# Attention stage of a fused attention, dense and routed layer: the weighted products of a pair of heads in one group per three jobs, one of three weight copies on ScalarE, keys loaded in three pieces and V in one

## The chip, the cores and the metric

The kernel runs on one core of a Trainium2 chip. The metric is the device time of one launch in microseconds (us), lower is better. The core has a matrix engine (TensorE, PE in the profile, with its weight loads as PEld), a vector engine (DVE), a scalar engine (ACT), a general engine (GpSimd, POOL) and SyncE (SP), which here only issues transfers. Each engine runs its own queue in order, and engines wait for each other through semaphores.

## What is computed

Three layers follow each other; only the first is touched.

```python
# q, k, v: (4, 8, 576, 64); window 64
scores = q @ k.T / sqrt(64);  keep only 0 <= row - col < 64
attn = softmax(scores)                       # exp(x - max) / sum
x = (attn @ v) laid out as (2304, 512)
xn = x / rms(x) * rms_g
y = (silu(xn @ w_gate) * (xn @ w_val)) @ w_out     # (512 -> 1536 -> 512)
# then each row goes to the best of 8 experts: relu(y @ w1[e]) @ w2[e], gated
```

## The kernel before

The attention is done in 16 units (`UNITS`), a unit being one pair of heads of one batch. A unit has nine blocks of 64 rows (`NBLK`), each against 128 keys, and they are done three at a time: a job is three blocks, a unit three jobs (b = 0, 1, 2), 48 jobs in all. The two heads of a pair lie side by side: each block's queries are laid out with zeros (`lay_out_q`, on GpSimd) so that one 128-row product makes the scores of both heads.

For job j the work passes through the engines as follows.

- TensorE, `scores`: one mask product (L922) and six score products recorded in L928 (two entries per product) into the bank of b. It waits until the exponentials of job j-3 are done, and at the first job of a unit for queries and keys.
- VectorE, `row_max` (L1262); ScalarE, `exps` (L692): three exponentials, each with its row sum read back; VectorE, `normalize` (L1270 reciprocal, L1272 product) of the job before.
- TensorE, `weights_T` (L945): three transposes of job j-3, into one of two banks in turn; VectorE, `copy_pt` (L1278), copies them to `pt`.
- TensorE, `weighted` (L957): for job j-4, 12 entries of L957 (three blocks, two heads) into one of two output banks in turn; ScalarE, `copy_o` (L702), copies them to `xo`.

So PE's queue holds, for each job: mask, scores, transposes, weighted products. DVE's: maximum, copy of transposes, normalize. ACT's: exponentials, copy of outputs.

SyncE's queue loads, unit by unit: `load_q` of unit n+2, the first piece of V of unit n, `load_k` of unit n+1 (it waits until all scores of unit n-1 are done), two more pieces of V, and `store_xT` of unit n-2, which waits for ScalarE's copies. A unit moves 288 KB each of q, k and output, and 512 KB of V, whose windows overlap. Beside it come strips of the dense weights (`load_dense` on ScalarE's queue before pairs 3, 5 and 7, 1 MB each).

GpSimd lays out the queries of the next unit and between them splits weight strips into a high and a low part, squares the first chunk of x (units 10 and 11), scales it (`scale_first`: quarters 0 and 1 at n = 14, quarters 2 and 3 at n = 15, after `lay_out_q(n)`) and splits it (`split_first`). The scale waits for the inverse roots, which go through ScalarE (`root_first`, with the table for square roots, then `copy_first_roots`, L765, after pair 6), VectorE (at jobs 1 and 2 of pair 6) and TensorE (`token_mean_squares` before unit 12, `spread_first_roots` in the last job of unit 13).

After job 47, `attention_end` mixes the last transposes and weighted products with the first gate products (`half_gate`, L1000 to L1002), which wait quarter by quarter for `split_first`. Then the dense stage runs, bound by TensorE.

```python
def job(j, i, u, b):                       # DVE, before
    row_max(j, u, b)
    copy_pt(*job_before(j, i, T_LAG))
    normalize(*job_before(j, i, 1))
```

Of the kernel before, what the change touches and what calls it, by code (L numbers as in the profile page):

```python
# [29 lines left out]
P = 128  # L30
# [11 lines left out]
T_LAG, O_LAG = 3, 4  # L42
# [79 lines left out]
def build(nc, qT, kT, vW, w_gate, w_val, w_out, rms_g, wg2, wg2T, w1, w2, out):  # L122
# [18 lines left out]
    with ExitStack() as ctx:  # L141
# [138 lines left out]
        k_in = [sem(f"k_in{u}") for u in range(2)]  # L280
        v_in = [[sem(f"v_in{u}_{b}") for b in range(JOBS)] for u in range(2)]
# [3 lines left out]
        q_first, k_first, qbd_first = sem("q_first"), sem("k_first"), sem("qbd_first")  # L285
# [24 lines left out]
        exp_ready, pt_copied, o_copied = sem("exp_ready"), sem("pt_copied"), sem("o_copied")  # L310
# [8 lines left out]
        def job_before(j, i, lag):  # L319

            i = (i - lag) % (2 * JOBS)
            return j - lag, i // JOBS, i % JOBS

        def windows(b):

            return slice(max(BPJ * b - 1, 0), BPJ * (b + 1) - 1)
# [30 lines left out]
        def _(sp):  # L357
            sp.dma_start(qraw[0][:, FIRST], qT[0][:, FIRST]).then_inc(q_first, 16)
            sp.dma_start(qraw[0][:, REST], qT[0][:, REST]).then_inc(q_in[0], 16)
            sp.dma_start(kt[0][:, REST], kT[0][:, REST]).then_inc(k_in[0], 16)  # L360
# [10 lines left out]
            def load_k(n, u):  # L371
                sp.wait_ge(s_ready, done(JOBS * (n - 1)))
                sp.dma_start(kt[u][:], kT[bass.ds(n, 1)].rearrange("a p s -> p (a s)")).then_inc(k_in[u], 16)

            def load_v(n, u, b):
                sp.wait_ge(o_ready, done(JOBS * (n - 2) + b + 1))
                sp.dma_start(vt[u][:, windows(b), :].rearrange("p j c -> p (j c)"),
                             vW[bass.ds(n, 1), :, windows(b), :].rearrange("a p j c -> p (a j c)")
                             ).then_inc(v_in[u][b], 16)

            def store_xT(n, u):
                sp.wait_ge(o_copied, done(JOBS * (n + 1)))
# [12 lines left out]
            load_k(1, 1)  # L395
            for u in range(2):
                for b in range(JOBS):
                    load_v(u, u, b)
            load_q(2, 0)
            load_q(3, 1)  # L400
            load_k(2, 0)

            def unit(n, u, q=True, k=True):
                if q:
                    load_q(n + 2, u)
                load_v(n, u, 0)
                if k:
                    load_k(n + 1, 1 - u)
                load_v(n, u, 1)
                load_v(n, u, 2)  # L410
                store_xT(n - 2, u)
# [13 lines left out]
            unit(UNITS - 1, 1, q=False, k=False)  # L425
            load_wo(1)
# [15 lines left out]
            sp.wait_ge(o_ready, done(STEPS))  # L442
# [1237 lines left out]
```

## Time and profile before

| | us |
|---|---|
| median of 3 runs (838.75 to 839.33) | 838.92 |
| the profiled execution | 838.17 |
| its span | 836.2 |
| attention, first work to first gate product of f = 1 | up to 105.6 |
| TensorE busy | 820.1 (98%) |
| VectorE busy | 484.2 |
| ScalarE busy | 287.1 |
| GpSimd busy | 211.9 |

The granted clock of TensorE is full in all 40 slices of the page. In the first five slices (104 us) VectorE is 6 to 8 tenths busy, ScalarE 5 to 7, and the DMA engines 7 to 9 tenths; after that TensorE is nearly alone.

### The profile page before, as it was taken

To read this page: it belongs to the slowest core of one execution; us is meant where nothing else is said; L and a number is where in the kernel's file an instruction comes from. 1 tells how busy PE (TensorE), PEld (TensorE's weight loads), DVE (VectorE), ACT (ScalarE), POOL (GpSimd) and SP (SyncE) were. 2 spreads that over 40 slices of the span, in tenths; PEclk is the share of its full clock that TensorE was granted. 3 is DMA by queue.
4 is the path that set the end of the run, shared out by engine and by line. 5 is a ranking of instruction groups with operands and counts; after the bars stand their busy time and mean duration, and the time that the engine had idled before them with its cause. 6 is when DMAs were issued, how large, how long until landed. Compare 5 with 4: busy or idle time off the path is not lost.

```text
span 836.2 us, 15281 instructions
## 1 busy us (share of the span) xinstructions
PE 820.1 (98%) x4809; PEld 732.6 (88%) x4810; DVE 484.2 (58%) x994; ACT 287.1 (34%) x665; POOL 211.9 (25%) x187
## 2 busy tenths in 40 slices
PE   8999999999999999999999999999999999999996
PEld 7888799999999998999999999998888888888885
DVE  7888632548675865676485767735224645564351
ACT  6777521321212121212213123334315435444340
POOL 4276899303002100300030000050831111111100
PEclk9999999999999999999999999999999999999999
DMA  7898970010002000200100012216354544646100
GB/s 233 266 312 273 326 303 1 1 44 33 1 1 76 0 1 4 76 0 1 55 22 1 1 39 101 101 39 225 96 208 151 189 175 151 225 180 216 53 17 23
DMA packets 38888, 88.24 MB, mean 106 GB/s; under 512 B 4063, under 2 KB 13791, under 8 KB 38305
## 3 DMA queue, kind: packets, MB, share of 16 engines
q1 hardware_dynamic: 33632, 72.79, 25.3%
q0 software_dynamic: 3360, 10.23, 3.4%
q10 hardware_dynamic: 1824, 4.31, 1.6%
q8 instruction: 40, 0.66, 0.3%
q14 instruction: 32, 0.25, 0.1%
HBM read 73.16 MB, written 14.94 MB: 105 GB/s over the span
## 4 chain that ended last, share of the span: by engine, by line
PE 95%; POOL 2%; DVE 1%; ACT 1%; issue 1%; DMA 1%; ACTq 0%; POOLq 0%; DVEq 0%
PE ps L1000 27%; PE ps L1002 27%; PE ps L1001 27%; PE ps L928 3%; PE ps L1138 2%; PE ps L957 2%; PE ps L922 2%; PE ps L945 1%; PE ps L1059 1%; ACT pr L692 1%; POOL xn_lo L551 0%; POOL xc L543 0%; PE ps L1175 0%; DVE nmax L1262 0%; PE ps L903 0%
## 5 line engine op out<-in xcount | busy, mean ns | idle before, releaser
L1000 PE MATMUL ps<-xn_hi,GV_hi 128*128 128x384 f32 x576 | 195.7, 340 | 1.1 <-POOL xn_lo L551 0.7
L1001 PE MATMUL ps<-xn_lo,GV_hi 128*128 128x384 f32 x576 | 193.0, 335 | 0.8 <-issue 0.8
L1002 PE MATMUL ps<-xn_hi,GV_lo 128*128 128x384 f32 x576 | 193.4, 336 | 0.0
L1000 PEld LDWEIGHTS ps<-xn_hi,GV_hi 128*128 128x128 f32 x576 | 108.2, 188 | 5.4 <-POOL xn_lo L551 1.0
L1001 PEld LDWEIGHTS ps<-xn_lo,GV_hi 128*128 128x128 f32 x576 | 108.2, 188 | 3.3
L1002 PEld LDWEIGHTS ps<-xn_hi,GV_lo 128*128 128x128 f32 x576 | 108.1, 188 | 0.9 <-issue 0.9
L1359 DVE CUSTOM_DVE_ANT_0 ps<-ysb,wrb 128x512 f32<-128x512 f32 x120 | 92.1, 768 | 6.0 <-ACT ysb L756 1.0
L743 ACT ACTIVATE sig<-ps 128x384 f32<-128x384 f32 x72 | 35.4, 492 | 168.7 <-PE ps L1002 168.6
L749 ACT ACTIVATE h_hi<-ps 128x384 fp32r<-128x384 f32 x72 | 35.4, 491 | 166.7 <-DVE ps L1329 166.7
L1002 PE MATMUL ps<-Wo_hi,h_lo 128*128 128x512 f32 x216 | 85.5, 396 | 0.0
L1001 PE MATMUL ps<-Wo_lo,h_hi 128*128 128x512 f32 x216 | 85.3, 395 | 0.0
L1324 DVE TENSOR_TENSOR silu<-sig,ps 128x384 f32<-128x384 f32 x72 | 39.8, 552 | 77.2 <-ACT sig L743 73.8
L1000 PE MATMUL ps<-Wo_hi,h_hi 128*128 128x512 f32 x216 | 84.1, 389 | 0.3 <-issue 0.3
L1000 PE MATMUL ps<-EW_hi,h2T_hi 128*128 (+1 forms) x168 | 67.2, 400 | 1.1 <-DVE osb L1564 1.1
L1000 PE MATMUL ps<-EW_hi,xsT_hi 128*128 (+1 forms) x168 | 68.0, 405 | 0.0
L626 POOL DMA_INDIRECT out<-osb,sidx x21 | 21.1, 1004 | 182.1 <-DVE osb L1564 181.6
L559 POOL TENSOR_TENSOR ssq<-xraw 128x384 f32<-128x384 f32 x5 | 5.6, 1115 | 240.5 <-DMA xraw<-xT_rows 240.5
L1002 PE MATMUL ps<-EW_hi,xsT_lo 128*128 (+1 forms) x168 | 66.5, 396 | 0.0
L1001 PE MATMUL ps<-EW_lo,xsT_hi 128*128 (+1 forms) x168 | 66.3, 395 | 0.0
L1329 DVE TENSOR_TENSOR ps<-silu,ps 128x384 f32<-128x384 f32 x72 | 40.5, 563 | 44.3 <-PE ps L1002 43.0
L1002 PE MATMUL ps<-EW_hi,h2T_lo 128*128 (+1 forms) x168 | 65.7, 391 | 0.0
L1001 PE MATMUL ps<-EW_lo,h2T_hi 128*128 (+1 forms) x168 | 65.7, 391 | 0.0
(176 smaller groups left out, 1393.2 us busy)
## 6 DMA issues: line engine op xcount, KB each, us to landing
EW_raw<-w SPq DMA_DIRECT2D x32, 1024.0 KB, 7.1
vt<-vW SPq DMA_DIRECT2D x32, 192.0 KB, 4.4
xT_rows<-xo SPq DMA_DIRECT2D x16, 288.0 KB, 4.0
y_rows<-ysb SPq DMA_DIRECT2D x6, 768.0 KB, 4.1
qraw<-qT SPq DMA_DIRECT2D x15, 288.0 KB, 4.0
kt<-kT SPq DMA_DIRECT2D x15, 288.0 KB, 4.7
xraw<-xT_rows SPq DMA_DIRECT2D x5, 768.0 KB, 5.6
vt<-vW SPq DMA_DIRECT2D x16, 128.0 KB, 4.3
```

Of the source, the lines that this page charges most:

```text
L626: nc.gpsimd.indirect_dma_start(out=out, out_offset=bass.IndirectOffsetOnAxis(ap=sidx[:, s:s + 1], axis=0), in_=osb[s % DEEP][:], in_offset ...
L743: nc.scalar.activation(sig[:], ps[:, G_BANK + f % 2, 0:CH], ACT.Sigmoid).then_inc(sig_ready, 1)
L749: nc.scalar.activation(h_hi[f % 2][:], ps[:, V_BANK + f % 2, 0:CH], ACT.Copy).then_inc(hi_ready, 1)
L922: return nc.tensor.matmul(ps[:, S_BANK + b, 0:BPJ * KEYS], ident_r[:], masks, start=start, stop=not start)
L928: last = nc.tensor.matmul(ps[:, S_BANK + b, i * KEYS:(i + 1) * KEYS], qbd[u][:, k, :], kt[u][:, k0:k0 + KEYS], start=(start and i == 0), s ...
L957: last = nc.tensor.matmul(ps[half, O_BANK + (JOBS * u + b) % 2, i * WIN:(i + 1) * WIN], vt[u][:, max(k - 1, 0), half], pt[:, b, i * P + a ...
L1000: nc.tensor.matmul(out, a_hi, b_hi, start=start, stop=False)
L1001: nc.tensor.matmul(out, a_hi, b_lo, start=False, stop=False)
L1002: return nc.tensor.matmul(out, a_lo, b_hi, start=False, stop=stop)
L1324: nc.vector.tensor_tensor(silu[:], sig[:], ps[:, G_BANK + f % 2, 0:CH], ALU.mult).then_inc(silu_ready, 1)
L1329: nc.vector.tensor_tensor(hid, silu[:], hid, ALU.mult).then_inc(h_ready, 1)
L1359: v.tensor_tensor_reduce(out=ps[:, MISC, :], in0=ysb[:, t, :], in1=wrb[:, e, :], scale=1.0, scalar=0.0, op0=ALU.mult, op1=ALU.add, accum_o ...
```

## The change

The order of work within a unit changes; no arithmetic does.

- `weighted` becomes one call per unit: 36 entries of L957 for unit n-2, in the first job of unit n, after the first transposes of unit n-1. It waits for all three copies of the transposes, for the V of the unit, and for `normalize` of job (n-1, 1).
- `weights_T` of unit n-1, job b is done in job b of unit n.
- Of the three copies of transposed weights, ScalarE makes the third (`move_pt`, ahead of the exponentials of b = 2). VectorE's two wait for the weighted products of the unit before.
- `copy_o` becomes one copy of 128x576 per unit, after the exponentials of b = 0.
- The reciprocals of b = 1 go to the second output bank; this `normalize` waits for `copy_o`, and the next `weighted` waits for this `normalize`.
- Keys come in three transfers per unit with a semaphore each, V in one. SyncE's order is q, three pieces of k, V, store. The first piece of k may start one job earlier.
- The third strip of dense weights is loaded by SyncE after the last unit's loads, no longer by ScalarE before pair 7.
- All four quarters of `scale_first` come at n = 15, after `lay_out_q(15)`. `attention_end` has a new order, and the last `normalize` uses another bank.

```diff
-T_LAG, O_LAG = 3, 4
+O_LAG = 2
@@ sync
-            def load_k(n, u):
-                sp.wait_ge(s_ready, done(JOBS * (n - 1)))
-            def load_v(n, u, b):
-                sp.wait_ge(o_ready, done(JOBS * (n - 2) + b + 1))
+            def load_k(n, u, b):
+                sp.wait_ge(s_ready, done(JOBS * (n - 2) + min(b + 2, JOBS)))
+            def load_v(n, u):
+                sp.wait_ge(o_ready, done(n - 1))
             def store_xT(n, u):
-                sp.wait_ge(o_copied, done(JOBS * (n + 1)))
+                sp.wait_ge(o_copied, done(n + 1))
...
+            load_strip(2)
             load_wo(1)
             load_strip(3)
@@ gpsimd
-            scale_at = {14: (0, 1), 15: (2, 3)}
+            scale_at = {15: range(KD)}
@@ scalar
+            def move_pt(n, u):
+                act.wait_ge(pt_ready, done(JOBS * n + JOBS))
+                act.wait_ge(o_ready, done(n))
+                nc.scalar.activation(pt[:, JOBS - 1, :], ps[:, T_BANK + (JOBS * u + JOBS - 1) % 2, 0:BPJ * P],
+                                     ACT.Copy).then_inc(pt_moved, 1)
+            def copy_o(n, u, stored):
+                act.wait_ge(o_ready, done(n + 1))
+                act.wait_ge(xT_out[u], stored)
+                nc.scalar.activation(xo[u][:], ps[:, O_BANK:O_BANK + 2, :].rearrange("p a c -> p (a c)")[:, 0:S],
+                                     ACT.Copy).then_inc(o_copied, 1)
...
+                for j, u, b in jobs(2 * JOBS * pair, 2 * JOBS):
+                    if b == JOBS - 1:
+                        move_pt(2 * pair + u - 1, 1 - u)
                     exps(j, u, b)
+                    if b == 0:
+                        copy_o(2 * pair + u - O_LAG, u, 16 * pair)
...
-            load_dense(2)
@@ tensor
+            def weighted(n, u, loads, normalized):
+                pe.wait_ge(pt_copied, done(2 * n + 2))
+                pe.wait_ge(pt_moved, done(n + 1))
+                pe.wait_ge(v_in[u], loads)
+                pe.wait_ge(o_copied, done(n))
+                pe.wait_ge(p_ready, normalized)
+                for k in range(NBLK):
...
+                    weights_T(n - 1, 1 - u, b)
+                    if b == 0:
+                        weighted(n - O_LAG, u, 16 * pair, done(JOBS * (n - 1) + 2))
...
             def attention_end(c, par):
+                weights_T(UNITS - 1, 1, 0)
+                pe.wait_ge(exp_ready, done(STEPS - JOBS + 1))
+                half_gate(c, 0, par, *gv_weights[0], range(0, 1))
+                weighted(UNITS - 2, 0, 8 * UNITS, done(STEPS - 1))
+                weights_T(UNITS - 1, 1, 1)
+                half_gate(c, 0, par, *gv_weights[0], range(1, KD))
+                weights_T(UNITS - 1, 1, 2)
                 pe.wait_ge(exp_ready, done(STEPS))
                 half_gate(c, 0, par, *gv_weights[1])
+                weighted(UNITS - 1, 1, 8 * UNITS, done(STEPS))
@@ vector
+            def normalize(n, u, b, bank=None):
+                j, blocks = JOBS * n + b, slice(b * BPJ, (b + 1) * BPJ)
+                if b == 1:
+                    dve.wait_ge(o_copied, done(n - 1))
+                    bank = O_BANK + 1
...
+            def normalize_last(n, u, b):
+                if b == 0:
+                    normalize(n - 1, 1 - u, JOBS - 1)
+                else:
+                    normalize(n, u, b - 1)
+            def copy_pt(n, u, b):
+                dve.wait_ge(pt_ready, done(JOBS * n + b + 1))
+                dve.wait_ge(o_ready, done(n))
...
+            def job(j, n, u, b):
                 row_max(j, u, b)
+                if b < JOBS - 1:
+                    copy_pt(n - 1, 1 - u, b)
+                normalize_last(n, u, b)
```

## Rows read from the trace of the kernel before

**Rows 1.** Page, part 1: busy time, share of the span, instructions.

```profile
PE 820.1 (98%) x4809; PEld 732.6 (88%) x4810; DVE 484.2 (58%) x994; ACT 287.1 (34%) x665; POOL 211.9 (25%) x187
```

**Rows 2.** Busy time by stretch: engines (instructions), PE clock, DMA share, GB/s.

```profile
30.50:36.10 5.60, 5.60 (x70) 4.89 (x66) 5.00 (x13) 4.13 (x22) 1.46 (x3) 1.00 0.84 262
41.70:47.50 5.80, 5.75 (x70) 4.89 (x66) 5.09 (x13) 4.21 (x22) 4.96 (x5) 1.00 1.02 376
```

**Rows 3.** Timeline of PE, unit 6: start, duration, engine, line, operation, count.

```profile
37.06 0.49 PE L945 MATMUL ps<-ident,pr 128*128 128x128 f32 x3
37.48 0.57 PE L957 MATMUL ps<-pt,vt 128*64 128x64 f32 x12
37.98 0.44 PE L922 MATMUL ps<-mask,ident_r 128*128 128x384 f32 x1
38.26 0.83 PE L928 MATMUL ps<-kt,qbd 128*128 128x128 f32 x6
```

**Rows 4.** Timeline of PE, jobs 3 and 4, before any weighted products.

```profile
8.83 0.42 PE L922 MATMUL ps<-mask,ident_r 128*128 128x384 f32 x1
...
10.00 0.42 PE L922 MATMUL ps<-mask,ident_r 128*128 128x384 f32 x1
```

**Rows 5.** Timeline of DVE, job 5, where it runs without a gap.

```profile
13.49 0.55 DVE L1262 TENSOR_REDUCE nmax<-ps 128x3 f32<-128x384 f32 x1
...
13.96 0.55 DVE L1278 COPY pt<-ps 128x384 f32<-128x384 f32 x1
...
14.42 0.17 DVE L1270 RECIPROCAL ps<-den 128x3 f32<-128x3 f32 x1
...
14.63 0.55 DVE L1272 TENSOR_TENSOR pr<-pr,ps 128x384 f32<-128x384 f32 x1
...
15.10 0.55 DVE L1262 TENSOR_REDUCE nmax<-ps 128x3 f32<-128x384 f32 x1
```

**Rows 6.** Timeline of ACT: exponentials of one job, its copies of 192 and 384 columns.

```profile
70.07 0.37 ACT L692 ACTIVATE pr<-ps,nmax 128x128 f32<-128x128 f32 x1 [0.49 <-DVE nmax L1262]
...
71.11 0.33 ACT L702 ACTIVATE xo<-ps 128x192 f32<-128x192 f32 x1
...
109.18 0.49 ACT L749 ACTIVATE h_hi<-ps 128x384 fp32r<-128x384 f32 x1 [1.29 <-DVE ps L1329]
```

**Rows 7.** Timeline of PE: first mask products of units 9 and 15, with idle time.

```profile
54.20 0.43 PE L922 MATMUL ps<-mask,ident_r 128*128 128x384 f32 x1 [1.03 <-ACT pr L692]
...
90.76 0.45 PE L922 MATMUL ps<-mask,ident_r 128*128 128x384 f32 x1 [0.52 <-POOL qbd L521]
```

**Rows 8.** Timeline of SP: issue of the keys of unit 9.

```profile
48.37 0.33 SPq L373 DMA_DIRECT2D kt<-kT  x1
```

**Rows 9.** Page, part 6: transfers, KB each, median us from issue to landing.

```profile
kt<-kT SPq DMA_DIRECT2D x15, 288.0 KB, 4.7
```

**Rows 10.** Timeline of PE before unit 12: the mean squares.

```profile
72.06 0.83 PE L910 MATMUL ps<-ones_r,ssq 128*128 128x1 f32 x6
```

**Rows 11.** Timeline of ACT in unit 12: first table load, next exponential.

```profile
73.33 1.28 ACT L760 ACT_TABLE_LOAD   x1
...
76.19 0.37 ACT L692 ACTIVATE pr<-ps,nmax 128x128 f32<-128x128 f32 x1
```

**Rows 12.** Timeline of ACT: the inverse roots copied out.

```profile
85.27 0.50 ACT L765 ACTIVATE ssq<-ps 128x384 f32<-128x384 f32 x1
```

**Rows 13.** Timeline of POOL after the roots: queries of unit 15, last split.

```profile
89.24 1.47 POOL L521 TENSOR_SCALAR qbd<-qraw,heads 128x576 f32<-128x576 f32 x2
...
99.27 1.00 POOL L551 TENSOR_TENSOR xn_lo<-xc,xn_hi 128x384 fp32r<-128x384 f32 x1
```

**Rows 14.** Timeline of PE: end of the attention, first gate product of f = 1.

```profile
100.33 0.45 PE L1000 MATMUL ps<-xn_hi,GV_hi 128*128 128x384 f32 x1 [0.69 <-POOL xn_lo L551]
...
105.14 0.57 PE L957 MATMUL ps<-pt,vt 128*64 128x64 f32 x12
105.64 0.45 PE L1000 MATMUL ps<-xn_hi,GV_hi 128*128 128x384 f32 x1
```

More of the change, by code:

```diff
@@ L394, in _ @@
             load_q(1, 1)
-            load_k(1, 1)
+            for b in range(JOBS):
+                load_k(1, 1, b)
             for u in range(2):
-                for b in range(JOBS):
-                    load_v(u, u, b)
+                load_v(u, u)
             load_q(2, 0)
             load_q(3, 1)
-            load_k(2, 0)
+            for b in range(JOBS):
+                load_k(2, 0, b)
             def unit(n, u, q=True, k=True):
@@ L405, in unit @@
                     load_q(n + 2, u)
-                load_v(n, u, 0)
                 if k:
-                    load_k(n + 1, 1 - u)
-                load_v(n, u, 1)
-                load_v(n, u, 2)
+                    for b in range(JOBS):
+                        load_k(n + 1, 1 - u, b)
+                load_v(n, u)
                 store_xT(n - 2, u)
@@ L771, in _ @@
             act.dma_start(raw_out[0][:].rearrange("p k d -> p (k d)"), w_out[0]).then_inc(wo_in[0], 16)
-            load_dense(2)
             with act.Fori(STRIP_PAIRS[2], UNITS // 2) as pair:
                 pair_of_units(pair)
-            for i in range(O_LAG):
-                copy_o(*job_before(STEPS + i, i, O_LAG), 16 * (UNITS // 2))
+            copy_o(UNITS - 2, 0, 8 * UNITS)
+            move_pt(UNITS - 1, 1)
+            copy_o(UNITS - 1, 1, 8 * UNITS)
             def round_part(e, i):
@@ L1004, in _, with half_gate @@
             gv_weights = ((0, G_BANK, g_ready), (1, V_BANK, v_ready))
-            def half_gate(c, f, par, kind, bank, ready):
+            def half_gate(c, f, par, kind, bank, ready, ks=range(KD)):
                 strip, cols = f // FPS, slice(f % FPS * P, (f % FPS + 1) * P)
-                for k in range(KD):
+                for k in ks:
                     if f == 0:
@@ L1012, in half_gate @@
                                  (xn_hi[par][:, k, :], xn_lo[par][:, k, :]), k == 0, k == KD - 1)
-                last.then_inc(ready, 1)
+                if ks[-1] == KD - 1:
+                    last.then_inc(ready, 1)
             def gate_val(c, f, par, between=None):
@@ L1027, in sum_y @@
                 if first and f == 0:
-                    pe.wait_ge(o_copied, done(STEPS))
+                    pe.wait_ge(o_copied, done(UNITS))
                 if f == 0:
@@ L1302, in _ @@
                                             sq[:, 0:TPC].unsqueeze(2).to_broadcast([P, TPC, P]), ALU.mult).then_inc(first_diag, 1)
-            for i in range(T_LAG):
-                copy_pt(*job_before(STEPS + i, i, T_LAG))
-                if i == 0:
-                    normalize(*job_before(STEPS, 0, 1))
+            dve.wait_ge(rrms_ready, done(1))
+            normalize(UNITS - 1, 1, JOBS - 1, MISC)
+            for b in range(JOBS - 1):
+                copy_pt(UNITS - 1, 1, b)
             def norm_rows(c, k, par):
```

116 lines of the change are left out of this document (41 added, 75 removed).

## The prediction

> **What bounds the kernel now.** I read the busy times first [rows 1]: PE is busy for 98% of the span, so time is saved only where PE's queue gets shorter or where PE waits. The change touches the attention alone, up to the first gate product of f = 1 at 105.64 [rows 14]; behind it nothing changes, and the dense stage needs GpSimd's weight strips some us before PE uses them, so what the attention gains is the kernel's gain. Second, busy time by stretch: in a quiet unit PE is busy in all of its 5.60 us, DVE in 5.00, ACT in 4.13 [rows 2]. So PE is the bound of a unit, DVE is close behind, and a change that lightens PE meets DVE next. Third, PE's timeline within a job [rows 3]: transposes at 37.06, weighted products at 37.48, mask at 37.98, scores at 38.26. A third of 5.60 is 1.87 a job. Last, the waits of PE: the first mask of unit 9 comes after 1.03 idle [rows 7], and there is a second like it at unit 11; the page names ACT, but those exponentials were long done, and it was the keys: issued at 48.37 [rows 8], they took up to 5.5 us to land, over their median of 4.7 [rows 9], behind a stretch with the DMA share at 1.02 and 376 GB/s [rows 2]. Unit 15 waits 0.52 for GpSimd's layout of queries [rows 7].
>
> **PE's own work after.** With its 12 weighted products a job takes 1.87. Without any, the masks of jobs 3 and 4 stand at 8.83 and 10.00 [rows 4]: 1.17. So a group of 12 costs 0.70. Its merged row is 0.57 long [rows 3], of which the last product is about 0.27, so the starts of 11 take 0.30: 0.028 for each. 12 x 0.028 = 0.34 is streaming, and 0.36 is the change over from transposes and to the mask. One group of 36 costs 36 x 0.028 + 0.36 = 1.37 where three cost 2.10. PE's unit falls from 5.60 to 2 x 1.17 + (1.17 + 1.37) = 4.88.
>
> **DVE's own work.** Where it runs without a gap [rows 5], the maximum takes 0.47 to the next start, the copy 0.46, reciprocal 0.21, product 0.47: 1.61 a job, 4.83 a unit. ACT takes one copy of three, so DVE has 4.37. ACT: exponentials 1.04 from first to the copy behind them [rows 6], three times 3.12; the copy of 384 columns took 0.49 and of 192 took 0.33 [rows 6], so one of 576 should take 0.65 (an estimate by these two); 3.12 + 0.49 + 0.65 = 4.26. By work alone PE would still be the bound, at 4.88.
>
> **The new wait.** But the products of unit n-2 (first job of unit n) wait for `normalize` of job (n-1, 1), and DVE's first copy in that job waits for the products. This closes a ring through both queues, once a unit. From the copy's start on DVE: copy 0.46, reciprocal 0.21, product 0.47 (job 2 of the unit before); maximum 0.47, copy 0.46, reciprocal 0.21, product 0.47 (b = 0); maximum 0.47, reciprocal 0.21, product to its end 0.56 (b = 1). That is 3.99 [rows 5]. Then PE: 0.06 from a release to a start (as from 100.27 to 100.33, [rows 13, 14]), 35 x 0.028 + 0.27 = 1.25 for the products, 0.05 to DVE. Sum 5.35. It is longer than PE's 4.88, so I take 5.35 as the unit: PE waits some 0.47 in front of the weighted products of each unit, and the gain per unit is 0.25, not 0.72. Only the maximum of b = 0 runs beside the products. Queued behind the waiting products is the mask of b = 1; behind DVE's waiting copy the whole rest of its unit.
> I walked the other queues past the ring, from the start W of the products: scores of b = 1 are ready at W + 2.29 and DVE wants them at 2.44; those exponentials end at 4.1 and their reciprocal comes at 4.53; `move_pt` ends by 4.6 and is wanted at 5.35. None is in the ring, the tightest has 0.15.
>
> **Up to the roots.** In job 5 the maximum starts at 13.49 in both; after, the reciprocal follows at once and its product ends at 13.49 + 0.47 + 0.21 + 0.56 = 14.73, so the first group of 36 starts at 14.79 in unit 2. Unit 13's starts 11 rings later: 14.79 + 58.85 = 73.6. Onto this come:
> - Table loads. From 73.33 to 76.19 [rows 11], 2.86 us, ACT does no exponentials. Before, this hid in ACT's slack. After, the exponentials of unit 11 end at W + 0.37, so those of (12, 0) start at 3.23, copy of outputs by 4.95, (12, 1) ends at 6.0, and the normalize in the ring starts at 6.05 and ends at 6.82 instead of 5.30: +1.5. Where this cover is partly there it costs nothing, at worst 2.9. The Trainium skill ("ScalarE: Activation LUTs", section What ACT_TABLE_LOAD costs) gives about 2.66 us for a switch to another set, drain included; the row's 2.86 holds two loads and a small root, so by the page's figure for both switches the cost would be up to 5.3. The trace decides for less.
> - Mean squares, up to 0.83 on PE [rows 10] before unit 12, and a like pair for the spread in unit 13: before both were paid in full, now 0.47 of each lies in PE's wait: +0.2 for the first; the second comes behind the roots' path in part.
> - Transfers. The first keys may be asked for 1.2 earlier and the other pieces are wanted 1 to 2 jobs later, while V, stored outputs and queries have 6 us and more. So the stalls of units 9 and 11 (1.0 each) and 0.2 at unit 8 should go. Bounds: 0 to 2.2 left; I take 0.5, since a unit's traffic (1.41 MB) is now spread over 5.35, and three units with strip and chunk (6.07 MB) at the 376 GB/s of [rows 2] need 16.1, just 3 x 5.35. A piece has 96 KB instead of 288, V 512 instead of three pieces: packets of a unit stay as many.
> Unit 13's products start at 73.6 + 1.5 + 0.2 + 0.5 = 75.8. The exponentials of (13, 2) end 5.7 later, the copy of the roots 0.5 after that: 82.1, where before it was 85.77 [rows 12]. Gain 3.7.
>
> **From the roots to the end.** GpSimd goes from 85.77 to 100.27 = 14.5 [rows 12, 13] without a gap, and this includes the layout of unit 15, 1.47 [rows 13] less a small overlap, now done before the roots: 13.1 is left, its last split ends at 95.2. PE reaches its last gate quarter at about 95.0, so the split stays last. From 100.27 to 105.64 [rows 13, 14] lie three groups of 12 and two of transposes; after there is one of transposes and one of 36: 3 x 0.50 + 0.42 go, about 1.15 comes, 5.37 - 0.8 = 4.6. Gate products of f = 1 at 99.8. Gain 105.64 - 99.8 = 5.8 to 5.9. Moving strip 2 to SP: GpSimd wants it only after its first split of w_out, which begins at 95.2; issued near 88, it has over 7 us before that even begins (288 KB take 4.7, [rows 9]). It costs 0.
>
> **Sum.** Profiled execution 838.17 - 5.9 = 832.3. The median of the runs is 0.75 above that execution: 833.0.
>
> **Rivals.**
> B. The ring doesn't bind, PE does (the release comes earlier than by my rows, or DVE pipelines its steps closer). 11 units at 4.88 instead of 5.35: 5.2 less, of which PE's insertions take 0.5: 828. For it: the margin is only 0.47 in 5.35. Against: every step of the ring is a row.
> C. Slower. The transfers become the bound. Place: units 6 to 14, 9 x 1.41 + 2.9 = 15.6 MB, hidden in 9 x 5.35 = 48 us at 324 GB/s. The quiet unit moved 262 at a share of 0.84, which is 312 at a full share: 50, costing 1.8. It decides from 15.6 MB / (48.2 + 5.9) = 288 GB/s on: below that all is lost. At 280 it is 55.7, 7.5 lost: 840.5. Against it: 376 was moved in one stretch. The Trainium skill ("DMA: Bandwidth & Descriptors", section Bandwidth) calls for transfers of 1 MiB and puts those under 64 KB down to descriptors; pieces of 96 KB go that way. By it C would gain weight; it changes no term above.
> D. The ring passes every disturbance on. Before, a late key, a table load or a late layout met slack in three queues; now each meets 0.15 to 0.5. If the 2.2 of key stalls stay and the table loads cost 2.9, the gain is 5.9 - 1.7 - 1.4 = 2.8: 836.
> E. The ring is longer than 5.35 and reaches 5.60 (0.25 more, for example by exponentials that come in late): 11 x 0.25 = 2.8 lost, with D's terms nothing is left: 839.
>
> **How the numbers follow.** Forecast 0.50, B 0.14, C 0.09, D 0.20, E 0.07. Its own range is 831 to 835. The range to hold 8 in 10 takes in B's edge and D: 828.0 to 837.8. A measurement here tells 0.2%, 1.7 us, from no change. Faster by more (below 837.2): the forecast, B and most of D, 0.81. Within it: E and the end of D, 0.09. Slower: C and a bad E, 0.10.
>
> **What would show it.** Right: L957 in 16 merged groups of 36 of about 1.25; mask to mask of b = 0 every 5.35 in quiet units; PE idle for 0.4 to 0.5 ahead of L957, released by DVE L1272's line; DVE idle in front of the copy of b = 0, released by L957; one longer unit of about 6.9 at unit 12 to 13, with ACT's table loads; no idle in front of the masks of units 9 and 11; POOL without a gap from the roots for 13.1. Wrong: units of 4.9 (B), units above 5.5 with the DMA share near 1 and keys or V released by DMA (C), POOL not ready.

## The result and the profile after

| us | before | after |
|---|---|---|
| median (lowest to highest) of 9 runs each | 838.75 (836.79 to 840.25) | 836.74 (834.96 to 837.63) |
| profiled execution, its span | 838.17, 836.2 | 836.86, 834.9 |
| first gate product of f = 1 | 105.64 | 104.76 |

The ratio is 0.9970, with an interval of 0.9959 to 0.9981: some 2.5 us faster, where 5.9 were forecast. A second, later set of 8 runs of the changed kernel gave 835.19 and a ratio of 0.9957 (0.9937 to 0.9976). So the change is a gain, but of 5.9 us only 2.5 to 3.6 arrived. In the profiled executions the attention gave 0.88, and the part behind it 0.42.

That small remainder hides two larger things. TensorE stops once near 330 us for a reason that the profile doesn't name ("issue"), and longer after the change. The second row of each pair is the same place of the program, the router's products, some 235 us later; first before, then after:

```profile
331.40 0.34 PE L1001 MATMUL ps<-xn_lo,GV_hi 128*128 128x384 f32 x1 [0.77 <-issue]
...
565.51 2.85 PE L1167 MATMUL ps<-wr,yT_last 128*128 128x8 f32 x24
```

```profile
330.79 0.33 PE L1005 MATMUL ps<-xn_hi,GV_lo 128*128 128x384 f32 x1 [1.51 <-issue]
...
565.83 2.85 PE L1171 MATMUL ps<-wr,yT_last 128*128 128x8 f32 x24
```

So there the changed kernel is 0.32 behind. What puts it 1.3 ahead at the end is, by the rows, a spell at half clock right behind these products, worth 1.7, that the profile of before has and that of after has not (last section). That the change gains rests on the two sets of runs, not on this pair of profiles.

The page of after: busy times, and two of the transfers (KB each, median us to landing):

```profile
PE 810.5 (97%) x4809; PEld 729.5 (87%) x4810; DVE 474.9 (57%) x978; ACT 291.3 (35%) x649; POOL 211.9 (25%) x187
...
vt<-vW SPq DMA_DIRECT2D x16, 512.0 KB, 4.8
...
kt<-kT SPq DMA_DIRECT2D x47, 96.0 KB, 4.1
```

PE's busy time fell by 9.6 us against [rows 1], much more than the span, which fell by 1.3: PE does less, and waits for most of what it saved. The timeline of PE in after, the group of 36 weighted products in the first job of units 2 to 13 (two quiet ones and unit 10 left out) (start, duration, idle time ahead and its releaser), shows where:

```profile
16.86 1.98 PE L967 MATMUL ps<-pt,vt 128*64 128x64 f32 x36
22.95 1.27 PE L967 MATMUL ps<-pt,vt 128*64 128x64 f32 x36 [0.38 <-DVE pr L1282]
28.31 1.27 PE L967 MATMUL ps<-pt,vt 128*64 128x64 f32 x36 [0.38 <-DVE pr L1282]
...
44.41 1.27 PE L967 MATMUL ps<-pt,vt 128*64 128x64 f32 x36 [0.38 <-DVE pr L1282]
51.08 1.27 PE L967 MATMUL ps<-pt,vt 128*64 128x64 f32 x36
57.69 1.27 PE L967 MATMUL ps<-pt,vt 128*64 128x64 f32 x36
...
68.42 1.27 PE L967 MATMUL ps<-pt,vt 128*64 128x64 f32 x36 [0.39 <-DVE pr L1282]
75.02 1.27 PE L967 MATMUL ps<-pt,vt 128*64 128x64 f32 x36
80.90 1.27 PE L967 MATMUL ps<-pt,vt 128*64 128x64 f32 x36 [0.89 <-DVE pr L1282]
```

Quiet units take 28.31 - 22.95 = 5.36, with 0.38 of waiting for the DVE product: that is the ring. But unit 2 starts late and its group lasts 1.98, and the groups of units 8, 9 and 12 come 6.67, 6.61 and 6.60 behind the ones ahead of them. What stands ahead of them on PE, in four stretches of the same timeline:

```profile
14.66 0.44 PE L925 MATMUL ps<-mask,ident_r 128*128 128x384 f32 x1 [1.93 <-POOL qbd L517]
...
49.72 0.43 PE L925 MATMUL ps<-mask,ident_r 128*128 128x384 f32 x1 [1.49 <-DMA kt<-kT]
...
56.33 0.44 PE L925 MATMUL ps<-mask,ident_r 128*128 128x384 f32 x1 [1.44 <-DMA kt<-kT]
...
73.68 0.41 PE L925 MATMUL ps<-mask,ident_r 128*128 128x384 f32 x1 [0.88 <-issue]
```

These are the first masks of units 2, 8, 9 and 12; such waits were forecast to go. The last three wait for keys (at 73.68 the profile names none; it goes when the keys come earlier, below). SyncE's queue in after, ahead of unit 8, tells why (start, duration of the issue), behind ScalarE's copy of outputs:

```profile
40.86 0.65 ACT L703 ACTIVATE xo<-ps 128x576 f32<-128x576 f32 x1
...
41.95 0.41 SPq L378 DMA_DIRECT2D xT_rows<-xo  x1
42.65 0.40 SPq L364 DMA_DIRECT2D qraw<-qT  x1
43.24 2.04 SPq L369 DMA_DIRECT2D kt<-kT  x3
```

The keys stand behind the store, and the store waits for ScalarE's copy of outputs, which now is one copy late in the job (40.86 to 41.51). So they are asked for at 43.24 and would be wanted at 49.72 - 1.49 = 48.23. Call this distance their lead, 5.0 here, and compare it with how long after the issue PE could start on them:

| first keys, us | before | after | `store_late` (below) |
|---|---|---|---|
| lead, units 5, 6, 7 | 5.6, 5.9, 5.7 | 4.8, 5.0, 4.8 | 6.3, 6.2, 6.3 |
| unit 8: lead, mask behind the issue | 6.1, no wait | 5.0, 6.5 | 6.5, 6.7 |
| unit 9 | 4.8, 5.8 | 5.5, 6.9 | 6.4, no wait |
| unit 11 | 5.4, 6.4 | 4.6, no wait | 6.3, no wait |
| unit 12 | 7.6, no wait | 5.4, 6.3 | 7.0, 7.3 |

The change was to bring the keys 1.2 earlier. Of the units in this table only unit 9 got more lead, 0.7; the others got 0.7 to 2.2 less. In units 8, 9 and 12 the keys then came 6.3 to 6.9 after their issue (before, the slowest of units 9 and 11 took 6.4), so a lead of 5.0 to 5.5 was not enough.

### The profile page after: what moved, and what is told of

Its sections match the earlier page's. It is cut to its first block, busy times and chain, and to the rows that moved or that the text cites. A ratio compares the mean times of both kernels' runs of the same rounds, so it can differ in the third digit from the quotient of the medians.

```text
span 834.9 us, 15300 instructions
## 1 busy us (share of the span) xinstructions
PE 810.5 (97%) x4809; PEld 729.5 (87%) x4810; DVE 474.9 (57%) x978; ACT 291.3 (35%) x649; POOL 211.9 (25%) x187
## 4 chain that ended last, share of the span: by engine, by line
PE 90%; DVE 3%; issue 3%; ACT 2%; DMA 1%; POOL 1%; SPq 0%; DVEq 0%; ACTq 0%; POOLq 0%
PE ps L1003 27%; PE ps L1005 27%; PE ps L1004 27%; PE ps L1142 2%; PE ps L967 2%; PE ps L1063 1%; ACT pr L688 1%; DVE nmax L1266 1%; DMA kt<-kT 1%; DVE pr L1282 1%; DVE pt L1295 1%; PE ps L931 1%; PE ps L1179 0%; DVE ps L1280 0%; PE ps L951 0%
```

## The experiments

The ratios are to the kernel before, run on the same chip, with 95% intervals; its medians there were 838.12 to 838.73. "Group of unit n" is the start of the 36 products that PE does in the first job of unit n. Each kernel has one profile, and two profiles of one kernel differ too (`after_again`, below), so the rows show where time goes and the ratios how much of it counts. Line numbers shift by a few from kernel to kernel.

### Order of SyncE's queue

`store_late`: the same transfers with the same waits, only that each store moves behind the queries and keys that stood behind it.

```diff
 def unit(n, u, q=True, k=True):
-    if q: load_q(n + 2, u)
-    if k: load_k(n + 1, 1 - u, b)      # three pieces
     load_v(n, u)
+    if q: load_q(n + 3, 1 - u)
+    if k: load_k(n + 2, u, b)          # three pieces
     store_xT(n - 2, u)
```

> The changed kernel with SyncE's order in a unit turned: V of n, queries of n+3, keys of n+2, and only then the store of unit n-2. The first keys no longer stand behind a store that waits for ScalarE's output copy. Theory SyncE order: keys are issued about 1.5 us earlier relative to their unit, the idle of PE ahead of the first masks of units 8, 9 and 12 (1.49, 1.44, 0.88) goes, the distances of 6.6 there fall to about 5.4, and the kernel gains 3 to 3.8 us. Rival (the DMA engines are simply full there): the landing moves with the load, units 8 and 9 keep over 1 us each, gain under 1 us.

Measured: 833.29 (832.68 to 834.26), ratio 0.9955 (0.9939 to 0.9972). SyncE and PE in store_late around unit 8:

```profile
40.19 2.01 SPq L369 DMA_DIRECT2D kt<-kT  x3
42.67 0.36 SPq L378 DMA_DIRECT2D xT_rows<-xo  x1
...
46.92 0.44 PE L930 MATMUL ps<-mask,ident_r 128*128 128x384 f32 x1 [0.26 <-DMA kt<-kT]
```

The keys of unit 8 are issued 6.5 ahead of their demand and still take 6.7, so it is the lead that helps, not a faster landing. The waits for keys are 0.26, 0.18 and 0.22 (units 8, 10 and 12) where they were 1.49, 1.44 and 0.88 (units 8, 9 and 12). The groups of units 8 and 9 come after 5.42 and 5.37. The place of the store was the cause of the waits. From unit 12 to 13 it now takes 6.55 where after had 5.88, so part of the gain is given back to the table loads, which the late keys had covered. By the ratio alone the edit can't be told from after (0.9970 and 0.9957): the 3 to 3.8 us that I expected are seen in the rows, not in the time.

`start_v1_late`: at the start, V of unit 1 is loaded behind the queries and keys of unit 2 instead of ahead of them.

```diff
-            for u in range(2):
-                load_v(u, u)
+            load_v(0, 0)
             load_q(2, 0)
             load_q(3, 1)
             for b in range(JOBS):
                 load_k(2, 0, b)
+            load_v(1, 1)
```

> The changed kernel, with the V of unit 1 (wanted at 20 us) issued after the queries of units 2 and 3 and the keys of unit 2. Theory start: the queries of unit 2, which landed at 12.9, land at about 11, PE's idle of 1.93 ahead of unit 2 and the slow clock behind it go, the first group of 36 starts near 14.8 instead of 16.86 and the second at 20.2 instead of 22.95: 2 to 2.8 us less. Rival (the queries were late for the total of bytes): the idle stays over 1 us, gain under 1 us.

Measured: 833.77 (833.06 to 836.44), ratio 0.9957 (0.9943 to 0.9972). GpSimd's layout of unit 2's queries, first in after, then in start_v1_late:

```profile
12.95 2.91 POOL L517 TENSOR_SCALAR qbd<-qraw,heads 128x576 f32<-128x576 f32 x4 [3.26 <-DMA qraw<-qT]
```

```profile
10.71 1.47 POOL L517 TENSOR_SCALAR qbd<-qraw,heads 128x576 f32<-128x576 f32 x2 [1.03 <-DMA qraw<-qT]
```

Both kernels issue these queries at the same time (5.85 and 5.84), but they land 2.2 earlier when no V of unit 1 is under way ahead of them. The first group starts at 14.93 (forecast 14.79; after 16.86). The waits at units 8, 9 and 12 stay (1.56, 0.60, 1.60). How much this is worth differs from execution to execution: in the eight profiles of kernels that issue as after does up to there, GpSimd starts this layout between 11.49 and 12.96 and the first group comes between 14.87 (`after_no_switch`) and 16.86 (after itself); in the four with V of unit 1 behind, it is 10.51 to 10.98 and 14.19 to 14.93. So the V ahead does hold the queries back, by 0.5 to 2.5, but the start in the profile of after is the latest of the eight, and the ratio doesn't tell this kernel from after.

`store_and_start`: both edits together.

> Both SyncE edits together: the store of unit n-2 behind the keys of unit n+2, and the V of unit 1 behind the keys of unit 2. By the traces of each alone (groups of 36 start 1.1 us earlier at unit 2 with the second, and lose 0.2 instead of 3.8 us at units 8, 9, 12 with the first), the last group should start near 98.4 and the time be 831 to 832.5, some 6 us below the kernel before: the size that was predicted for the change. Rival: the start is lost again in the full stretch, 833.

Measured: 832.24 (831.58 to 833.86), ratio 0.9917 (0.9896 to 0.9938). Groups of units 2, 3, 11, 12 and 13, and the first gate product of f = 1 in store_and_start:

```profile
14.64 1.27 PE L972 MATMUL ps<-pt,vt 128*64 128x64 f32 x36 [0.52 <-DVE pr L1287]
20.00 1.27 PE L972 MATMUL ps<-pt,vt 128*64 128x64 f32 x36 [0.38 <-DVE pr L1287]
...
62.91 1.27 PE L972 MATMUL ps<-pt,vt 128*64 128x64 f32 x36 [0.38 <-DVE pr L1287]
68.49 1.27 PE L972 MATMUL ps<-pt,vt 128*64 128x64 f32 x36
75.39 1.27 PE L972 MATMUL ps<-pt,vt 128*64 128x64 f32 x36 [1.05 <-DVE pr L1287]
...
99.28 0.45 PE L1008 MATMUL ps<-xn_hi,GV_hi 128*128 128x384 f32 x1
```

The ratio is clear of that of after in the first set of runs (0.9959 to 0.9981) and touches that of the second (0.9937 to 0.9976). This is the timeline that was forecast: a start at 14.64 (14.79), units of 5.36 (5.35), 5.58 over the mean squares (+0.2), 6.90 over the table loads (6.9), unit 13 at 75.39 (75.8) and the gate at 99.28 (99.8). The forecast time was 833.0. (Of the 6.4 gained over before at that place 0.8 is lost again up to the router's products, most of it at the stop near 330, which is 1.20 long here.)

### The ring

`rden_sbuf_free`: the reciprocals are written over the row sums in SBUF instead of into a PSUM bank, so that neither VectorE nor the weighted products need the waits that protect the bank.

```diff
-                if b == 1:
-                    dve.wait_ge(o_copied, done(n - 1))
...
-                rden = ps[:, bank, RDEN_AT:RDEN_AT + BPJ]
+                rden = den[u][:, blocks]
...
-                pe.wait_ge(p_ready, normalized)
```

> The changed kernel, with the reciprocals of the row sums written over the row sums in SBUF instead of into a PSUM bank; the wait of the weighted products for `normalize` and that of `normalize` for the output copy are gone. Theory ring: in quiet units the distance of two groups of 36 weighted products falls from 5.37 to PE's own 4.88, about 0.45 per unit in 8 or 9 undisturbed units, so 3 to 4 us less than the changed kernel, if no keys are later for it. Rival (DVE's own work or late transfers bound the unit): 5.2 to 5.4 stays, within 0.5 us of the changed kernel. If the operand in SBUF made DVE's product slower or faster than 0.56, the rows will show it.

Measured: 840.56 (838.44 to 842.90), ratio 1.0041 (1.0016 to 1.0066): slower. The ring is open, since groups come every 4.91 (15.38, 20.30, 25.22, 30.13, 35.04) with no wait ahead of them, and PE's own 4.88 of the forecast is right. But new costs come. GpSimd and VectorE in rden_sbuf_free, two layouts with the product of `normalize` beside them:

```profile
28.86 2.21 POOL L517 TENSOR_SCALAR qbd<-qraw,heads 128x576 f32<-128x576 f32 x2 [2.69 <-PE ps L931]
...
28.81 0.56 DVE L1276 TENSOR_TENSOR pr<-pr,den 128x384 f32<-128x384 f32 x1
...
29.96 0.59 DVE L1276 TENSOR_TENSOR pr<-pr,den 128x384 f32<-128x384 f32 x1
```

The pair of layouts takes 2.21, where it took 1.47. And the next keys don't hold the pace: the mask of unit 7 waits 1.35 for them at 40.20. The larger cost comes from unit 7 on, where GpSimd splits weight strips beside the units: VectorE's product is held until GpSimd's instruction is over. GpSimd and VectorE in rden_sbuf_free:

```profile
66.59 2.54 POOL L527 TENSOR_TENSOR GV_lo<-GV_raw,GV_hi 128x1024 fp32r<-128x1024 f32 x1
...
67.96 1.59 DVE L1276 TENSOR_TENSOR pr<-pr,den 128x384 f32<-128x384 f32 x1
```

The 48 products take 852 ns on average where they take 554 in after, 14.3 us of DVE in all, and PE's transposes wait 4.8 for them. The group of unit 13 comes at 79.16, only 1.7 before that of after, and 2.65 of lead had been there at unit 3 (20.30 against 22.95). I expected 3 to 4 us less than after; it is slower than before.

`rden_sbuf_wait`: the same, but the wait of the weighted products for `normalize` stays.

> As the kernel before it in this list, but the weighted products still wait for `normalize` of the job (n-1, 1), though nothing needs it. It parts the wait from the place of the reciprocals. Theory ring: the distance stays at 5.37 and the time at that of the changed kernel, within 0.5 us. Rival (the place in PSUM was the cost): 4.9, as without the wait.

Measured: 842.61 (841.51 to 844.42), ratio 1.0070 (1.0052 to 1.0088). The period is 5.39 again (15.29, 20.68, 26.07, 31.45, 36.84), with 0.40 idle released by the DVE product. It is the wait that makes the ring, not the place of the reciprocals. The place costs time all the same: I expected the time of after within 0.5, and it is some 6 slower, with the same held products (747 ns on average).

`ring_open`: the reciprocals of b = 1 go to another PSUM bank (`MISC`, unused up to unit 11), and up to there the weighted products don't wait for `normalize`.

```diff
-                if b == 1:
+                if b == 1 and early[0]:
+                    bank = MISC
+                elif b == 1:
                     dve.wait_ge(o_copied, done(n - 1))
                     bank = O_BANK + 1
...
-                pe.wait_ge(p_ready, normalized)
+                if normalized is not None:
+                    pe.wait_ge(p_ready, normalized)
...
+            pe.wait_ge(p_ready, done(2 * JOBS * MS_PAIR - 1))
             token_mean_squares()
```

> The changed kernel with the reciprocals of b = 1 in the bank MISC up to unit 11, where nobody else uses it, so that neither `normalize` nor the weighted products wait there; the operand stays in PSUM, unlike in the two kernels with it in SBUF. Theory ring: the distance is 4.9 in units 2 to 6, with GpSimd's layout at its old 0.74 per instruction, not 1.11. From unit 7 on the keys are later by what was gained (they stand behind the store), so PE waits over 2 us for them in places and most of the gain is lost: 0 to 2 us less than the changed kernel. Rival (ring was the cost): 3 us less or more.

Measured: 836.10 (832.08 to 840.16), ratio 0.9964 (0.9943 to 0.9985), the same as after. Groups come every 4.91 (22.07, 26.98, 31.90, 36.81), and the layouts take 1.47. Then PE in ring_open meets what comes next:

```profile
41.99 0.43 PE L925 MATMUL ps<-mask,ident_r 128*128 128x384 f32 x1 [1.36 <-POOL qbd L517]
...
55.47 0.44 PE L925 MATMUL ps<-mask,ident_r 128*128 128x384 f32 x1 [2.24 <-ACT pr L688]
```

In after's order of SyncE's queue a shorter unit only reaches the late transfers sooner. The edit has a cost of its own too: the last line of the cut hands the bank back, and PE waits 1.56 there, at 73.58. Unit 13 is at 81.53, later than after's 80.90.

`ring_open_all`: the ring open and both edits of SyncE's order.

> Ring open up to unit 11, and both SyncE edits. Theory, transfers bind next: ten units at 4.9 instead of 5.37 would give 4 to 4.7 us over the two SyncE edits alone, but 6.07 MB in units 6 to 8 need 16.1 us at the 376 GB/s seen, so those stay near 5.4; 1.5 to 3 us less than the two edits alone, 829 to 830.5. Rival (transfers hide): 827.5. Rival (it collides with GpSimd's strips or the roots): no gain, 832.

> Ring open up to unit 11 and both SyncE edits, the same kernel again: 830 to 831.5, a ratio of 0.990 to 0.992 to the kernel before.

Measured: 830.81 (830.37 to 833.15), ratio 0.9904 (0.9883 to 0.9925); on another chip 831.62 (829.72 to 832.29), ratio 0.9921 (0.9903 to 0.9939). It is the fastest kernel of the study, 7 to 8 us below before and 4 to 6 below after. Its waits, on PE in ring_open_all:

```profile
43.15 0.43 PE L930 MATMUL ps<-mask,ident_r 128*128 128x384 f32 x1 [0.59 <-ACT pr L693]
...
53.90 0.44 PE L930 MATMUL ps<-mask,ident_r 128*128 128x384 f32 x1 [0.67 <-DMA kt<-kT]
...
65.54 0.83 PE L918 MATMUL ps<-ones_r,ssq 128*128 128x1 f32 x6 [1.56 <-DVE pr L1293]
```

Its group of unit 11 is at 60.18, 2.7 ahead of that of store_and_start, and seven of the units up to there take 4.91 or 4.92. The last wait, in front of the mean squares, is where my edit hands the bank back; it costs most of what unit 12 had gained (67.58 against 68.49), but the table loads hide behind it, and unit 13 is 2.2 ahead (73.17 against 75.39). By the medians the ring was worth 1.4 us (832.24 to 830.81) once the transfers came in time, with intervals that overlap (0.9896 to 0.9938 and 0.9883 to 0.9925); in the rows it is 2.2 at unit 13. I had expected 1.5 to 3.

### Table loads

`after_no_switch` and `before_no_switch`: the square root of the mean squares is replaced by an exponential, in after and in before, so that ScalarE loads no other table. Both kernels leave out the right root.

```diff
-                nc.scalar.activation(sq[:, 0:TPC], ps[:, MISC, 0:TPC], ACT.Sqrt, bias=eps[:],
+                nc.scalar.activation(sq[:, 0:TPC], ps[:, MISC, 0:TPC], ACT.Exp, bias=eps[:],
```

> The changed kernel with an exponential in place of the square root of the first chunk, so that ScalarE loads no other table in unit 12; this leaves the right root out, so the first chunk's scale is not that of the reference. Table loads of 2.86 us. Theory of the prediction (loads cost 1.5 us in the ring): with the keys of unit 12 late besides, the group of unit 13 comes 5.37 after that of unit 12 instead of 5.88; 0.5 to 1.5 us less than the changed kernel. Rival (ScalarE's slack hides them): same within 0.3.

> The kernel before with an exponential in place of the square root of the first chunk, so without the two table loads; the right root is left out. Theory: before, ScalarE's slack hid them, so the time stays within 0.5 us of the kernel before. Rival (they cost as in the ring): 1 to 1.5 us faster.

Measured: 834.56 (833.69 to 840.99), ratio 0.9958 (0.9930 to 0.9985), and 838.90 (836.95 to 842.57), ratio 1.0010 (0.9993 to 1.0026). From the group of unit 12 to that of 13 it takes 5.59 in after_no_switch instead of after's 5.88. But start_v1_late, which has the loads, takes 5.59 too. So where PE has waited for keys and the exponentials are ahead, the loads cost 0 to 0.3, and the time can't be told from after's. In store_and_start, where the keys are in time, this unit takes 6.90, 1.3 over the 5.59; that the loads are the cause there is argued from the rows, as no run takes them out of that kernel. Before they cost nothing that can be seen. ACT in after:

```profile
74.26 1.28 ACT L763 ACT_TABLE_LOAD   x1
75.56 0.26 ACT L763 ACTIVATE sq<-ps,eps 128x3 f32<-128x3 f32 x1
75.84 1.28 ACT L688 ACT_TABLE_LOAD   x1
77.13 0.37 ACT L688 ACTIVATE pr<-ps,nmax 128x128 f32<-128x128 f32 x1
```

Two switches with the root between take 2.87, as they did before [rows 11]. By the Trainium skill ("ScalarE: Activation LUTs", section What ACT_TABLE_LOAD costs) each would be 2.66, 1.38 of it drain; these rows show its 1.28 for the load, and no drain: the next instruction starts 0.02 behind its end.

### Size of the pieces

`keys_one`: after, with the keys of a unit in one transfer, which waits as before the change until all three jobs of the unit two before are scored. `v_three`: after, with V in three transfers. `v_three_keys_one`: both.

```diff
# keys_one
-                sp.dma_start(kt[u][:, job_cols(b)], kT[bass.ds(n, 1), :, job_cols(b)]...)
+                if b == 0:
+                    sp.wait_ge(s_ready, done(JOBS * (n - 1)))
+                    sp.dma_start(kt[u][:], kT[bass.ds(n, 1)]...)
# v_three
-                sp.dma_start(vt[u][:]..., vW[bass.ds(n, 1)]...)
+                for b in range(JOBS):
+                    js = slice(max(BPJ * b - 1, 0), BPJ * (b + 1) - 1)
+                    sp.dma_start(vt[u][:, js, :]..., vW[bass.ds(n, 1), :, js, :]...)
```

> The changed kernel with the keys of a unit in one transfer from unit 1 on, which waits until unit n-1 is scored and which the first scores of a unit wait for. It tells what the three pieces are worth. Theory: SyncE reaches the keys only behind the store anyway, so the earlier wait of the first piece is worth nothing, but a piece of 96 KB lands before 288 KB do: with one transfer PE idles longer ahead of units 8, 9 and 12 by 0 to 0.7 each, 0.5 to 1.5 us slower than the changed kernel. Rival (pieces cost more issue time and smaller packets than they bring): equal or faster by up to 1.

> The changed kernel with V in three transfers as before, still waiting for the group of 36 of unit n-2. Theory (one V of 512 KB holds back what is issued behind it): the queries of unit 2 land near 11 again, PE's idle ahead of unit 2 is under 0.6, and the first group of 36 starts at 14.8 to 15.2. Rival (the pieces of V do not matter, the place in the queue does): 14.9 to 16.9 as in the changed kernel, and PE's idle of 0.5 to 1.5 at units 8, 9 and 12 as there.

> V in three and the keys in one transfer, all transfers as before but for what they wait for. If pieces matter at the start, here the queries of unit 2 land at 10.7 to 11. If not, the start is as late as with keys in one alone, 15.2, and the time 835 as there.

Measured: keys_one 835.04 (833.49 to 839.99), ratio 0.9963 (0.9946 to 0.9981); v_three 840.89 (838.23 to 845.70), 1.0041 (1.0017 to 1.0064); v_three_keys_one 837.55 (835.38 to 846.44), 0.9993 (0.9968 to 1.0019).

keys_one equals after, against my expectation of 0.5 to 1.5 slower: three pieces of keys are worth nothing that can be measured, though the last is wanted two jobs after the first. V in one transfer, on the other hand, matters: with V in three the kernel is slower than before. With keys in one besides, the loss is smaller (0.9993), and its interval overlaps that of keys_one. SyncE at the start of v_three and PE's longest wait there:

```profile
4.61 2.80 SPq L375 DMA_DIRECT2D vt<-vW  x6
7.46 0.90 SPq L364 DMA_DIRECT2D qraw<-qT  x2
...
58.05 0.43 PE L927 MATMUL ps<-mask,ident_r 128*128 128x384 f32 x1 [3.29 <-DMA kt<-kT]
```

Six issues of V take 2.80 of SyncE's queue, where two took 0.91 (4.61 to 5.52), and all that stands behind them is that much later. I had expected the queries to land near 11, as the sizes go; they landed at 13.61. The Trainium skill ("DMA: Bandwidth & Descriptors", section Bandwidth) calls for large transfers. v_three agrees with it in direction; for keys of 96 KB against 288 no difference shows. Which of the two counts more for v_three, bytes under way or time in the queue, these runs don't separate.

### Place of the scale

`scale_split`: after, with quarters 0 and 1 of `scale_first` ahead of the layout of unit 15 again, as before.

```diff
-            scale_at = {15: range(KD)}
+            scale_at = {14: (0, 1), 15: (2, 3)}
```

> The changed kernel with the first two quarters of `scale_first` back at unit 14, ahead of the layout of unit 15. In the changed kernel GpSimd waits 1.44 for the roots after that layout. Theory: the layout of 1.47 stands in the path again, so the last split and the end of the attention come 1.4 later, and unit 15 may wait for its queries: 1.4 to 2.4 us slower than the changed kernel. Rival (PE is later than the splits at the end): within 0.5.

Measured: 837.21 (834.70 to 842.56), ratio 0.9993 (0.9970 to 1.0016). The layout comes at 87.35, behind two quarters, and PE in scale_split waits for it:

```profile
88.87 0.44 PE L925 MATMUL ps<-mask,ident_r 128*128 128x384 f32 x1 [2.02 <-POOL qbd L517]
```

From the group of unit 13 to the first gate product of f = 1 it takes 25.33 where after takes 23.86, so the new place is worth 1.5 in the rows. By the medians it is 2 against after on the same chip (837.21 and 835.19, `after_again`) and 0.5 against the first set of after (836.74). The intervals overlap in both cases; the wait itself is in the row, and after has none there.

`after_again`: the changed kernel unaltered.

> The changed kernel itself once more, for its start. In its first profile the queries of unit 2 landed at 12.9 and PE's clock was granted at half for 3.4 us behind the idle time; the first group of 36 started at 16.86. In the kernel without table loads, whose start is the same code, it started at 14.87. Theory: the start is at the edge and differs from execution to execution by up to 2 us; this profile shows a start between 14.8 and 17, and the keys of units 8, 9 and 12 late again by 0.5 to 1.5 each. Rival: the start is always 16.9.

Measured: 835.19 (833.24 to 837.13), ratio 0.9957 (0.9937 to 0.9976). Its waits for keys are 0.82, 0.73 and 1.51, its first group is at 16.55. The late start and the three waits come again, with other sizes. Not in every execution: the same start code gave a first group at 14.87 in after_no_switch and 15.15 in scale_split.

## Why the prediction was right on the ring and wrong on the transfers

In the profiled execution the miss at the first gate product (104.76 instead of 99.8) lies ahead of the group of unit 13, at 80.90 instead of 75.8. Behind it, roots, splits and the end of the attention took 23.86 (80.90 to 104.76) where 24.0 were forecast.

| up to unit 13's group, us | forecast | after | store_and_start |
|---|---|---|---|
| start of unit 2's group | 14.79 | 16.86 | 14.64 |
| first unit behind it, over 5.35 | 0 | 0.74 | 0.01 |
| quiet units | 5.35 | 5.36 | 5.36 |
| stalls for keys, units 8, 9, 12 (forecast: in all) | 0.5 | 1.31, 1.25, 1.0 | under 0.1 |
| mean squares | 0.2 | 0.2 | 0.2 |
| unit 12 to 13 (table loads), over 5.36 | 1.5 | 0.52 | 1.54 |
| unit 13's group | 75.8 | 80.90 | 75.39 |

- **Right: the ring.** Forecast 5.35 and a wait of 0.47; measured 5.36 and 0.38. rden_sbuf_free and ring_open take the wait away and show PE's own 4.91 (forecast 4.88). Rivals B and E are out.
- **Right: the small terms.** The copy of 576 columns takes 0.65, the tail from roots to last split 12.9 (13.1), the end from there 4.40 (4.6), mean squares 0.2. Moving strip 2 to SyncE's queue shows no cost, though not for the reason given: it has 1 MB and not 288 KB, and was issued at 94.45 and not near 88, but GpSimd wants it only at 106.87. The table loads were about right (1.3 to 1.5) where nothing covers them, and I didn't see that late keys would.
- **Wrong: the transfers.** The step that failed is "the first keys may be asked for 1.2 earlier", with 0.5 for what is left. It read the semaphore of the keys alone. It didn't walk SyncE's queue past the changed order: the keys' turn comes behind a store that waits for a copy which the change makes once a unit and late. The keys' lead fell in units 5 to 8 from 5.6 to 6.1 down to 4.8 to 5.0, and was 5.0, 5.5 and 5.4 in units 8, 9 and 12, whose keys took 6.3 to 6.9 (the prediction had "up to 5.5" for the ones before; its own rows 7 and 8 give 54.20 - 48.37 = 5.8). Price 3.6 instead of 0.5; store_late, with leads of 6.2 and more from unit 5 on, takes nearly all of these waits away.
- **Wrong: the start.** I took 14.79 from DVE's queue, as if the queries of unit 2 landed when they did before. V of unit 1 is now one transfer of 512 KB in front of them, and they land at 12.95. In this execution it costs 2.1, and 0.7 more for the slow stretch behind it (below); in others the first group came at 14.87 to 16.55. With V behind, it came at 14.93 at the latest. Why the same V in three pieces ahead of the same queries did no harm before is not settled: v_three has the pieces back and is later still, v_three_keys_one is early (first group at 14.89) and stalls later.
- **Wrong: "what the attention gains is the kernel's gain".** 0.3 is lost at a stop of PE at 109.81 (0.60 where before has 0.28) and 0.9 more up to the router's products at 565, most of it at the stop near 330. store_late and store_and_start lose 1.0 and 0.8 of what they had gained over before, up to the same place. The profile names no releaser, and the cause stays open.
- **The rivals.** D named the right kind of event, a ring that passes every disturbance on, with a gain of 2.8, close to what came; but it put 2.9 on the table loads and left the stalls of units 9 and 11 as they were. The price was on the transfers and the start. C's bandwidth bound is out: store_and_start moves the same bytes and never waits for keys.

With both orders mended the forecast's own sum comes true: 832.24 against 833.0. A part of this is luck: the attention ends 0.5 ahead of the forecast there, and the dense stage loses 0.8, which the sum had at nothing.

## What to carry to other kernels

When a change moves a wait or merges work into one late step, follow every in-order queue on which that step releases something, the queue that only issues transfers too: a load doesn't start when its own semaphore allows it, but when the entries ahead of it have had theirs. Put what waits longest (a store) behind what is wanted soonest (the next loads). And before opening a ring that bounds a stage, look at what is next: here it was worth nothing until the loads came in time, and about 1.4 us after.

## What the runs showed of the hardware that was not expected

**GpSimd beside VectorE.** The layout on GpSimd (input and output in SBUF) takes 0.74 alone or beside a DVE product with one operand in PSUM, and 1.11 beside the same product with both operands in SBUF. What differs is where the reciprocals lie, the product's second operand. It goes the other way too: the product of 67.96, shown with `rden_sbuf_free`, ends at 69.55, 0.42 behind the GpSimd instruction that ends at 69.13, and a product that starts with a GpSimd instruction at 65.47 takes 1.45 and ends 0.41 behind it. In after, with the operand in PSUM, all 48 products take 0.55 beside the same splits. The Trainium skill ("SBUF — State Buffer", section SBUF: two separate sides) says that of a VectorE operation with two SBUF inputs and a GpSimd operation that reads SBUF the one that starts first shuts the other out for its whole instruction. The held products agree with it; the layouts agree in direction, with 0.74 lost per pair beside products of 0.56 and 0.59.

**The granted clock behind waits.** Busy time by stretch in after (PE, PEld, DVE, ACT, POOL, then PE's granted clock, DMA share and GB/s):

```profile
15.00:18.50 3.50, 3.50 (x40) 3.17 (x40) 0.56 (x1) 1.56 (x9) 0.86 (x2) 0.51 0.74 175
18.50:20.00 1.50, 1.50 (x23) 1.43 (x19) 1.07 (x3) 0.65 (x1) 0.00 (x0) 1.00 0.09 22
```

Behind the idle 1.93 at the start the clock is 1.2 GHz instead of 2.4 for some 3.4 us, and the group of 36 lasts 1.98 instead of 1.27. ring_open shows it twice, behind 1.73 and 2.24 of idle (groups of 2.19 and 2.07). It doesn't always follow: in scale_split a wait of 2.02 and in start_v1_late one of 1.60 did not bring it. In after it turned 2.1 of lateness into 2.8.

**The same once more in the dense stage.** Two stretches of 2 us in before, then the same two in after:

```profile
568.00:570.00 2.00, 2.00 (x9) 1.60 (x9) 0.91 (x5) 0.22 (x1) 0.00 (x0) 0.61 1.02 414
570.00:572.00 2.00, 2.00 (x7) 1.57 (x6) 0.00 (x0) 0.00 (x0) 0.00 (x0) 0.54 1.00 400
```

```profile
568.00:570.00 2.00, 2.00 (x14) 1.76 (x14) 0.91 (x5) 0.28 (x2) 0.00 (x0) 1.00 1.04 424
570.00:572.00 2.00, 2.00 (x11) 1.71 (x10) 0.23 (x2) 0.45 (x1) 0.00 (x0) 1.00 1.00 407
```

PE is busy in all of the time, and its clock is 1.2 GHz in most of these 4 us in before and 2.4 in after. Over 564 to 580 the mean is 0.89 in before; over 16 us, 0.11 is 1.7 us. The spell comes right behind the router's small products (24 of 128x8 in 2.85 us, shown in the first section) and moves with them: they end at 560.87 in ring_open_all, and from 561 to 562 the clock there is 0.50. It is there in nine of the seventeen profiles (both of before, and among the others those of store_and_start, rden_sbuf_free and ring_open_all) and not in eight (both of after, store_late and start_v1_late among them). It isn't tied to any edit that I can name, and it is as large as the 0.2% that a measurement here can tell: with one profiled execution of each kernel, part of a difference between two spans may be this alone. The page's slices of 21 us give no more than "90% or more" there, so "full in all 40 slices", said of before ahead of the prediction, was too much.
